# Attention units at every one and a half steps, unit 8's scores ahead, and block means copied by a transfer

## What is computed

```python
# local attention with block summaries, batch 2, 8 heads, 768 positions, head size 64
k_sum = k.reshape(B, H, nb, 32, D).max(axis=3)
v_sum = v.reshape(B, H, nb, 32, D).mean(axis=3)
scores = concat(window scores within 16 positions, q @ k_sum.T * scale + log(32))
attn_out = softmax(scores) @ concat(v, v_sum)
x = attn_out.transpose(0, 2, 1, 3).reshape(1536, 512)
# first MLP, 512 -> 2048 -> 512
h = np.maximum(x @ w_in, 0.0)
y = h * h @ w_out
# second MLP, 512 -> 1024 -> 512
h = y @ w2_in
solu = h * softmax(h)
out = ((solu - mean(solu)) / sqrt(var(solu) + 1e-6) * g_ln) @ w2_out
```

## Time and profile before

| what | before |
| --- | --- |
| median of 3 runs | 503.57 us (503.56 to 504.85) |
| the profiled execution's own time | 503.61 us |
| its span | 501.8 us |
| TensorE matmul busy | 486.9 us |
| VectorE busy | 249.9 us |
| ACT busy | 210.2 us |
| POOL busy | 50.0 us |
| mean granted TensorE clock over the span | 0.993 |

### The profile page before, as it was taken

The page is one execution under the profiler, slowest core; times in us unless marked ns, Lnnn a source line. Parts: engine busy times, 40 slices in busy tenths (PEclk is TensorE's granted clock), DMA queues, the critical chain, the costliest instruction groups (busy, mean ns, idle before and its releaser), DMA issues.

```text
span 501.8 us, 8265 instructions
## 1 busy us (share of the span) xinstructions
PE 486.9 (97%) x3144; PEld 439.3 (88%) x3144; DVE 249.9 (50%) x497; ACT 210.2 (42%) x549; POOL 50.0 (10%) x75
## 2 busy tenths in 40 slices
PE   8986999998999999999999999999999999999997
PEld 6765989898999999989999999999888888888885
DVE  4865556778644444454444243445854444444440
ACT  2854656655533344443433333333443333333331
POOL 2232333340200000000000000000000000000000
PEclk9997999999999999999999999999999999999999
DMA  8997023321310100041000032121222000000101
GB/s 297 327 361 243 21 72 112 94 69 33 133 35 20 41 21 22 20 150 37 21 0 1 13 116 84 43 84 45 82 68 74 29 21 22 21 22 21 38 26 42
DMA packets 26678, 37.38 MB, mean 74 GB/s; under 512 B 2480, under 2 KB 16592, under 8 KB 26640
## 3 DMA queue, kind: packets, MB, share of 16 engines
q1 hardware_dynamic: 25808, 34.60, 21.6%
q10 hardware_dynamic: 832, 2.27, 1.3%
HBM read 30.41 MB, written 6.29 MB: 73 GB/s over the span
## 4 chain that ended last, share of the span: by engine, by line
PE 90%; DVE 5%; issue 2%; ACT 2%; POOL 0%; DVEq 0%; ACTq 0%; POOLq 0%
PE bank L846 27%; PE bank L873 24%; PE bank L992 12%; PE bank L965 12%; PE bank L788 5%; PE bank L801 3%; PE bank L835 2%; PE bank L980 2%; PE bank L882 1%; ACT probs L425 1%; PE bank L812 1%; DVE k_sum L588 1%; DVE probs L627 1%; DVE solu L745 1%; DVE probs L612 1%
## 5 line engine op out<-in xcount | busy, mean ns | idle before, releaser
L846 PE MATMUL bank<-x_hi,win_hi 128*128 128x384 f32 x256 | 89.5, 350 | 0.0
L640 DVE TENSOR_TENSOR sqr<-relu 128x384 f32<-128x384 f32 x64 | 37.6, 587 | 98.9 <-ACT relu L479 98.7
L846 PE MATMUL bank<-x_lo,win_hi 128*128 128x384 f32 x256 | 86.3, 337 | 0.0
L846 PE MATMUL bank<-x_hi,win_lo 128*128 128x384 f32 x256 | 86.3, 337 | 0.0
L873 PE MATMUL bank<-h_hi,wout_lo 128*128 128x384 f32 x256 | 85.6, 334 | 0.0
L873 PE MATMUL bank<-h_hi,wout_hi 128*128 128x384 f32 x256 | 85.5, 334 | 0.0
L873 PE MATMUL bank<-h_lo,wout_hi 128*128 128x384 f32 x256 | 85.5, 334 | 0.0
L479 ACT ACTIVATE relu<-bank 128x384 f32<-128x384 f32 x64 | 31.5, 492 | 112.9 <-PE bank L846 112.9
L846 PEld LDWEIGHTS bank<-x_hi,win_hi 128*128 128x128 f32 x256 | 48.5, 190 | 4.1 <-issue 3.3
L846 PEld LDWEIGHTS bank<-x_lo,win_hi 128*128 128x128 f32 x256 | 48.7, 190 | 0.0
L846 PEld LDWEIGHTS bank<-x_hi,win_lo 128*128 128x128 f32 x256 | 48.6, 190 | 0.0
(11 more groups left out here) (79 smaller groups left out, 739.3 us busy)
## 6 DMA issues: line engine op xcount, KB each, us to landing
win_raw<-w_in_t SPq DMA_DIRECT2D x8, 512.0 KB, 12.2
wout_raw<-w_out_t SPq DMA_DIRECT2D x8, 512.0 KB, 12.9
win_raw<-w_t SPq DMA_DIRECT2D x8, 512.0 KB, 3.4
v_ext<-vwin SPq DMA_DIRECT2D x24, 144.0 KB, 2.4
out<-o_sb SPq DMA_DIRECT2D x12, 256.0 KB, 2.0
k_raw<-kT SPq DMA_DIRECT2D x7, 400.0 KB, 4.4
q_sb<-qT SPq DMA_DIRECT2D x24, 96.0 KB, 1.9
v_next<-vblk SPq DMA_DIRECT2D x4, 384.0 KB, 4.2
```

The costliest lines, as they stand in the source:

```text
L640: nc.vector.tensor_tensor(sqr[:, n % 3, :], relu[:, n % 2, :], relu[:, n % 2, :], ALU.mult)\
L846: last = nc.tensor.matmul(up_bank(n), win[a][:, f * WC + k * P:f * WC + (k + 1) * P], x[b][:, c % 2, k * CH:(k + 1) * CH], start=(k == 0 a ...
```

## The change

Three things are changed.

1. Rows 0 to 23 of `v_ext` are filled by a transfer on SP's queue (24 rows of 6 KB, SBUF to SBUF), after the first `load_vn` and ahead of the last five weight groups, with a wait on `vmean_ok`. The copy on POOL goes. `values(8)` to `values(15)` wait for the transfer's semaphore `vkept_in`.
2. Ahead of the loop, `scores(8)` stands right behind `scores(7)`; `turned(8)` and `scores(9)` come ahead of the loop, and slot 0 goes. ACT, VectorE and POOL follow: `exps(8)`, `maxima(8)`, `normalise(8)` sooner, unit 9's and 10's windows of keys ahead of `w_in_low(2)` and `w_in_low(3)`.
3. `SLOTS` counts half-steps. The slots of chunk 0 are at half-steps 2, 5, 8, 11, 14, 17, 20 and 23. An even half-step stands ahead of `up(n + 2)`, an odd one between `up(n + 2)` and `down(n)`. ACT and VectorE do `hidden(n + 2)` ahead of an odd slot's work and behind an even slot's. From unit 16 on the slots stand where they stood.

```diff
--- before.py
+++ after.py
@@ -57,19 +57,19 @@
 WG = 2
 
 
-SLOTS = {0: (None, 8, 9), 2: (8, 9, 10), 4: (9, 10, 11), 5: (10, 11, 12), 7: (11, 12, 13), 9: (12, 13, 14),
-         10: (13, 14, 15), 12: (14, 15, 16), 13: (15, 16, 17)}
+
+SLOTS = {3 * _u - 22: (_u, _u + 1, _u + 2) for _u in range(UPC, 2 * UPC)}
 for _u in range(2 * UPC, UNITS):
-    SLOTS[2 * (_u - UPC)] = (_u, _u + 1 if _u + 1 < UNITS else None, _u + 2 if _u + 2 < UNITS else None)
-
-
-def x_step(u):
-
-    n = next(n for n, group in SLOTS.items() if group[0] == u)
-    return n + 1 if u % UPC == 0 and u >= 2 * UPC else n
-
-
-X_AT = {x_step(u): u for u in range(UPC, UNITS)}
+    SLOTS[4 * (_u - UPC)] = (_u, _u + 1 if _u + 1 < UNITS else None, _u + 2 if _u + 2 < UNITS else None)
+
+
+def x_half(u):
+
+    h = next(h for h, group in SLOTS.items() if group[0] == u)
+    return h + 2 if u % UPC == 0 and u >= 2 * UPC else h
+
+
+X_AT = {x_half(u): u for u in range(UPC, UNITS)}
 
 V_AT = {6: 0, 8: 1, 10: 2, 12: 3}
 
@@ -166,7 +166,7 @@
 
         kwin_ok, ksum_ok, kbc_ok = sem("kwin_ok"), sem("ksum_ok"), sem("kbc_ok")
         vmean_ps, vmean_ok, vsum_ok, vavg_ok = sem("vmean_ps"), sem("vmean_ok"), sem("vsum_ok"), sem("vavg_ok")
-        vkept_ok = sem("vkept_ok")
+        vkept_in = sem("vkept_in")
         scores_ok, masked_ok, max_ok, exp_ok = sem("scores_ok"), sem("masked_ok"), sem("max_ok"), sem("exp_ok")
         den_ok, rec_ok, norm_ok = sem("den_ok"), sem("rec_ok"), sem("norm_ok")
         probsT_ps, probsT_ok, attn_ps = sem("probsT_ps"), sem("probsT_ok"), sem("attn_ps")
@@ -301,6 +301,9 @@
                 load_w(wout_raw, w_out_t, g - 1, wout_in)
                 if g == 5:
                     load_vn(0)
+                    sp.wait_ge(vmean_ok, PPB)
+                    sp.dma_start(v_ext[0:NB, :, :], v_ext_first[0:NB, 0, :].rearrange("p (j d) -> p j d", j=PPB))\
+                      .then_inc(vkept_in, 16)
             load_w(wout_raw, w_out_t, F1 // WG - 1, wout_in)
 
             for u in range(UPC, UNITS):
@@ -392,18 +395,17 @@
             windows_k(7)
             w_in_low(1)
             windows_k(UPC)
-            pool.wait_ge(vmean_ok, PPB)
-            nc.gpsimd.tensor_copy(v_ext[0:NB, :, :], v_ext_first[0:NB, 0, :].rearrange("p (j d) -> p j d", j=PPB))\
-              .then_inc(vkept_ok, 1)
+            windows_k(UPC + 1)
             w_in_low(2)
+            windows_k(UPC + 2)
             w_in_low(3)
-            windows_k(UPC + 1)
             for n in range(LAST):
-                if n in SLOTS and SLOTS[n][2] is not None and SLOTS[n][2] + 1 < UNITS:
-                    u = SLOTS[n][2] + 1
-                    if UPB <= u < UPB + PPB:
-                        summaries_k(1, u - UPB)
-                    windows_k(u)
+                for h in (2 * n, 2 * n + 1):
+                    if h in SLOTS and SLOTS[h][2] is not None and SLOTS[h][2] + 1 < UNITS:
+                        u = SLOTS[h][2] + 1
+                        if UPB <= u < UPB + PPB:
+                            summaries_k(1, u - UPB)
+                        windows_k(u)
                 if n + 4 < F1:
                     w_in_low(n + 4)
 
@@ -522,27 +524,32 @@
             x_high(5)
             copy_probsT(7)
             x_high(6)
-            w_out_high(0)
+            exps(8)
             x_high(7)
             w_in_high(2)
-            exps(8)
+            w_out_high(0)
+            copy_probsT(8)
             hidden(0)
+            copy_last(8)
             w_in_high(3)
+            hidden(1)
+            exps(9)
             w_out_high(1)
-            hidden(1)
             for n in range(STEPS):
                 if n % F1 == 0 and n:
                     chunk_y(n // F1 - 1)
-                if n in SLOTS and SLOTS[n][1] is not None:
-                    copy_probsT(SLOTS[n][1])
-                if n in X_AT:
-                    x_high(X_AT[n])
-                if n in SLOTS and SLOTS[n][1] is not None:
-                    copy_last(SLOTS[n][1])
-                if n + 2 < STEPS:
-                    hidden(n + 2)
-                if n in SLOTS and SLOTS[n][2] is not None:
-                    exps(SLOTS[n][2])
+                for h in (2 * n, 2 * n + 1):
+                    if h % 2 and n + 2 < STEPS:
+                        hidden(n + 2)
+                    if h in SLOTS and SLOTS[h][1] is not None:
+                        copy_probsT(SLOTS[h][1])
+                    if h in X_AT:
+                        x_high(X_AT[h])
+                    if h in SLOTS and SLOTS[h][1] is not None:
+                        copy_last(SLOTS[h][1])
+                for h in (2 * n, 2 * n + 1):
+                    if h in SLOTS and SLOTS[h][2] is not None:
+                        exps(SLOTS[h][2])
                 if n + 2 < F1:
                     w_out_high(n + 2)
                 if n + 4 < F1:
@@ -694,27 +701,32 @@
             x_low(4)
             normalise(7)
             x_low(5)
+            maxima(8)
             x_low(6)
+            normalise(8)
+            x_low(7)
             w_out_low(0)
-            x_low(7)
-            maxima(8)
-            normalise(8)
             hidden(0)
+            maxima(9)
+            hidden(1)
+            normalise(9)
             w_out_low(1)
-            hidden(1)
             for n in range(STEPS):
                 if n % F1 == 0 and n:
                     chunk_y(n // F1 - 1)
-                if n in SLOTS and SLOTS[n][2] is not None:
-                    maxima(SLOTS[n][2])
-                if n in X_AT:
-                    x_low(X_AT[n])
-                if n + 2 < STEPS:
-                    hidden(n + 2)
-                if n in SLOTS and SLOTS[n][2] is not None:
-                    normalise(SLOTS[n][2])
-                if n - 1 in SLOTS and SLOTS[n - 1][2] is not None and UPB <= SLOTS[n - 1][2] + 2 < UPB + PPB:
-                    sums_k(1, SLOTS[n - 1][2] + 2 - UPB)
+                for h in (2 * n, 2 * n + 1):
+                    if h % 2 and n + 2 < STEPS:
+                        hidden(n + 2)
+                    if h in SLOTS and SLOTS[h][2] is not None:
+                        maxima(SLOTS[h][2])
+                    if h in X_AT:
+                        x_low(X_AT[h])
+                for h in (2 * n, 2 * n + 1):
+                    if h in SLOTS and SLOTS[h][2] is not None:
+                        normalise(SLOTS[h][2])
+                for h in (2 * n - 2, 2 * n - 1):
+                    if h in SLOTS and SLOTS[h][2] is not None and UPB <= SLOTS[h][2] + 2 < UPB + PPB:
+                        sums_k(1, SLOTS[h][2] + 2 - UPB)
                 if n in V_AT:
                     sums_v(V_AT[n])
                     if V_AT[n] == VP - 1:
@@ -820,7 +832,7 @@
                     pe.wait_ge(vmean_ok, p + 1)
                 elif u < UPB:
                     pe.wait_ge(vw_in[p], 16 * (row - HPC + 1))
-                    pe.wait_ge(vkept_ok, 1)
+                    pe.wait_ge(vkept_in, 16)
                 else:
                     pe.wait_ge(vw_in[p], 16 * (row - HPC + 1))
                     pe.wait_ge(vs_in[p], 16)
@@ -906,6 +918,7 @@
             turned(4)
             turned(5)
             scores(7)
+            scores(8)
             values(3)
             values(4)
             values(5)
@@ -916,23 +929,26 @@
             up(1, range(0, 1))
             up(0, range(1, 2))
             values(7)
+            up(0, range(2, 3))
             up(1, range(1, 2))
-            up(0, range(2, 3))
-            scores(8)
+            turned(8)
+            up(0, range(3, 4))
+            scores(9)
             up(1, range(2, 3))
-            up(0, range(3, 4))
             up(1, range(3, 4))
             for n in range(STEPS - 2):
-                if n in SLOTS:
-                    a, b, c = SLOTS[n]
-                    if a is not None:
+                for j in (2 * n, 2 * n + 1):
+                    if j in SLOTS:
+                        a, b, c = SLOTS[j]
                         values(a)
-                    if b is not None:
-                        turned(b)
-                    if c is not None:
-                        scores(c)
-                up(n + 2)
-                down(n)
+                        if b is not None:
+                            turned(b)
+                        if c is not None:
+                            scores(c)
+                    if j % 2 == 0:
+                        up(n + 2)
+                    else:
+                        down(n)
 
             w2 = (win_hi, win_lo)
             ln = (lnT_hi, lnT_lo)
```

## The result

| kernel | median (us) | lowest to highest | runs |
| --- | --- | --- | --- |
| before | 503.56 | 502.32 to 504.85 | 6 |
| the change | 497.31 | 495.30 to 498.50 | 6 |

The change takes 0.9873 of the time of before, 95% interval 0.9843 to 0.9903: 6.3 us faster, 4.9 to 7.9 by the interval. The forecast was 494.2 with a range of 492.5 to 498.0, so the time is inside it, at its slow side: two thirds of the 9.4 us came. The profiled execution took 497.89 us, span 496.1.

The account below looks back on a forecast made before the run. TensorE, busy 97% of the span, was taken as the bound, with 11.9 us of idle and slow clock as the ceiling. Head 6.7 + loop 2.7 = 9.4 us off 503.6 gave 494.2, range 492.5 to 498.0.

Parts of the forecast that it names:

- Head: New order around units 6 to 9, ahead of and early in the loop: fewer waits and no slow clock, 6.7 us off.
- the walk: New head order timed with old trace durations: 7.5 us gained, less 0.5 for waits at `values(8)` and `turned(9)`, 7.0.
- the ledger: Head counted by losses: 9.2 us lost before, less new waits of 2.75, gives 6.4 us.
- Loop: Slots one and a half steps apart remove three waits of `turned` between 54 and 123 us: 2.7 us off.
- part 1: Section on the loop's slot spacing: 1.4 us to spare per slot where 0.7 was short; 2.7 us off.
- The transfer: Means issued by SP at 31.1, landing at 43.7; its wait at `values(8)` and that of `turned(9)` overlap, 0.5 us.
- rival 2: Head: 24-row transfer takes 2.0 us, not 0.4; `values(8)` waits 2.0; time 495.7 (about 494.6 at 0.9 us); chance 0.12.
- Rival 5: Transfer of the means lands far later, holding `values(8)`; slower than before past 53.1 us, 506 at 55; chance 0.04.
- The means' copy on POOL: Head: with this copy gone, the first instruction of `normalise(6)` takes 0.16 us where it took 1.12.
- Rival 3: Clock falls in the head after TensorE's idle at 26.5 to 31 us; 2.5 to 3.5 us, 496.9 to 497.7; chance 0.12.
- Rivals 1 and 4: 1: loop keeps its waits, 496.9, chance 0.08; 4: wait moves to `x_low(7)` or `turned(9)`, halving head gain, 497.5, chance 0.08.
- Signs: Trace marks of being right: `up(2)` near 39 us, full clock 38 to 50, no `turned` waits, step 14's up near 113.

Follow-up runs that it names:

- head_only: The change's head and transfer, with the slots of chunk 0 at their old steps; 496.44 us, ratio 0.9848 to the kernel before.
- low_first_early: The change with `w_in_low(15)` first on POOL at step 11 and the transfer issued one weight group sooner; 493.36 us, ratio 0.9784 to before.
- loop_only: The change's new slots with the old head, slot 0 and the means' copy on POOL; 505.19 us, ratio 1.0012 to before.
- low_first: The change with `w_in_low(15)` ahead of the slot's copies on POOL at step 11; 494.82 us, ratio 0.9826 to before.
- again: The changed kernel, unedited, measured a second time; 498.11 us, ratio 0.9894 to before.
- values3_first: low_first_early with `scores(8)` behind `values(3)` instead of ahead of it; 492.65 us, ratio 0.9771 to before.
- fill: The change with five matmuls on the idle tile between `scores(7)` and `scores(8)`; 496.80 us, ratio 0.9869 to before.
- pool_copy: The change with the copy of the means back on POOL and no transfer; 496.51 us, ratio 0.9851 to before.
- low_first_early_2: The low_first_early kernel measured again, unedited; 493.61 us, ratio 0.9789 to before.
- low_first_pool: The change with the edits of low_first and pool_copy together; 494.06 us, ratio 0.9803 to before.
- values3_first_pool: values3_first with the means copied by POOL instead of the transfer; 492.64 us, ratio 0.9771 to before.

## Why the prediction was right in the main and where it failed

- **Head, 6.7 us forecast.** Right in mechanism, and a little low: **head_only** is 7.6 us under before. There `values(8)` comes too late to meet the transfer, so the figure to compare is the walk without that wait, 7.5. The forecast took 0.5 off for the transfer and went 0.3 towards the ledger (6.4). In the trace of **low_first_early**, where nothing of the head is disturbed, each time is within 0.2 us of the walk: `turned(8)` 36.13 for 36.0, `scores(9)` 37.14 for 37.05, `values(8)` 43.32 for 43.2.
- **Loop, 2.7 us forecast.** The three waits went as said. The step that failed is the sentence on POOL in part 1: "POOL's `summaries_k(1,0)` then runs about 6 us after the slot began, `scores(16)` wants it at 9.2." It asked when the summary is wanted and not what is queued behind it. Two slots further, at step 11, `w_in_low(15)` is, and `up(15)` wants it at step 13. In the old order no slot stands at step 11. Measured: 2.0 us of wait in every trace of the new slots with the old place of `w_in_low(15)`, and in two of these five (the change, **loop_only**) 1.8 of low clock behind it. In **loop_only** that ate the whole gain of the slots. With `w_in_low(15)` first they give their 2.7 (**low_first_early** against **head_only**).
- **The transfer, 0.5 us forecast for its wait, 1.5 more by rival 2.** It lay between: no wait in the first trace, 0.53 in **low_first**, and 2.03 in **again**, which is rival 2's figure. SP's issue time differs (31.16, 31.35, 32.09), and so does the clock in the head. What the forecast took as fixed (issue at 31.1, due at 43.2) left no room. Issued nearly 4 us sooner it costs nothing. Rival 5, far later, did not come.
- **The means' copy on POOL.** The prediction counted 0.96 us as saved on `row_den`. That happens in the changed order even with the copy, and in the order of **values3_first**, where the collision is back, it costs 0.07 us. The item should have been zero for the transfer.
- **Rival 3, the clock.** It fell at 30 us in one of the two profiled executions of the change, and in that of **loop_only** too (0.52), so it is not of the new order alone. Of the eleven executions of the change six had a mean clock of 0.993 to 0.997, so falls are common, though the mean does not say where they stood. The price was put at 2.5 to 3.5 us; in the first trace it is 0.9 us (`scores(8)` to `turned(8)` 9.13 against 8.25), part of the slow stretch lying over time in which TensorE waits at full clock (0.67 us of the four from 30 to 34 in **again**). The clock behind the wait at step 13 cost twice that, and no rival named it. By its own sum the rival's lower time is 494.2 + 2.5 = 496.7, not 496.9; and rival 2's last figure, for 0.9 us in place of 0.4, is 494.7, not 494.6.
- **Rivals 1 and 4.** Their times, 496.9 and 497.5, are near the measured 497.31, and neither happened: no `turned` waits in the loop, and there is no wait at the last up part of hidden tile 0 or at `turned(9)`. The time alone could not have told them from what did.
- **Signs.** No clock under 1.00 between 38 and 50 us, no wait of `turned`, the first `row_den` at 0.16: these came in. `up(2)` starts at 39.73, 0.7 late by the clock. Step 14's up at 117.59 in place of 113 was the one that told of the loss; in **low_first_early** it starts at 112.93.
- **Sum.** The first trace's span is 4.5 us over that of **low_first_early**: 2.0 + 1.8 for `w_in_low(15)` and the clock behind it, 0.9 for the clock in the head, less 0.2 by which `scores(8)` starts earlier. With both faults mended and nothing else, the change gives 504.01 - 493.36 = 10.6 us, or 10.3 by the spans, close to the walk's 7.5 and the loop's 2.7; the forecast had 9.4 and called 11.9 the ceiling. That the time fell inside the stated range is in part luck: the range was widened for rivals that did not come, and the loss that filled it was in none of them.

What stays open: how much of what **fill** gained is the clock kept up. Its eight executions without a fall speak for an effect, but no trace of it shows a fall avoided, and between the profiled executions the difference is where the transfer landed. Why the same kernel's clock falls in one execution and not in the next is open too.

## What to carry to other kernels

When a producer is moved in an in-order queue, list every instruction that stands behind it, and ask of each when its reader is due; a wait that is harmless for its own consumer can hold a stranger two entries later. Put work whose inputs are ready ahead of work that waits for another engine. A transfer that is wanted within half a microsecond of its landing can cost time and make spread (here up to 2.0 us, and 2.7 us between executions): issue it as soon as its source is ready, or leave the copy where it is if the trace shows no path through the engine that it relieves.

## What the hardware showed beyond that

- A stop of 2.0 us at full work had two results in two executions of the same kernel: a granted clock of 0.50 and an up of 3.92 us behind it in one, 1.00 throughout in the other. The same for the gaps between 26 and 30 us. So what a stop costs in clock differs from execution to execution.
- The 24-row transfer seems to slow the queue beyond its 144 KB. From 38 to 44 us **head_only** (with it) moved 180, 205 and 317 GB/s, **pool_copy** (without) 237, 288 and 386: (57 + 83 + 69) GB/s x 2 us = 0.42 MB less, 1.1 us at the full 385, though its own bytes are counted. Two other pairs, from 34 to 44 us, have 0.46 MB (**low_first_early_2** and **low_first_pool**) and 0.22 MB less (**values3_first** and **values3_first_pool**), 1.2 and 0.6 us. With its own 0.4 us the transfer costs the queue an estimated 1.0 to 1.6 us. The forecast's first value was 0.4 us in all, its rival 2.0. The Trainium skill (SBUF — State Buffer, "Door 1: The DMA port swizzle") gives six of 16 ports for such a shape, an estimated 0.9 us; the traces agree in kind, at a somewhat larger figure.
